# Grams, the product with the state, and the outputs of a delta-rule attention, issued by 32 stationary columns instead of 64

## The reference, cut to what matters

```
k_n = k / (norm(k) + 1e-6)            # B, H, S, D = 4, 8, 768, 48
for t in range(S):
    y[t]  = q[t] @ state
    v_old = state^T k_n[t]
    state = state + beta[t] * outer(k_n[t], v[t] - v_old)
x = y as (3072, 384)
h  = ((x @ w1) * (x @ w2)) @ w3 @ w_out     # inner width 1024
e  = h @ w_in                               # 384 -> 1024
s  = e * softmax(e);  out = layernorm(s) * g_ln @ w_out2
```

## Time and profile before

| | |
|---|---|
| time, median of 3 runs | 772.83 us (772.46 to 775.34) |
| time of the profiled execution | 774.38 us |
| its span, first to last instruction | 772.7 us |
| PE busy | 741.6 us (96%) |
| PEld / DVE / ACT / POOL busy | 664.5 / 451.2 / 339.5 / 66.6 us |
| granted TensorE clock | 0.999 of full speed |

### The profile page before, as it was taken

One profiled execution on the slowest core, in us unless ns is written; L12 is line 12 of the kernel. 1 busy time (PEld: TensorE's weight loads), 2 busy tenths in 40 slices (PEclk: granted clock), 3 DMA queues, 4 the chain that ended last, 5 costly groups with the idle time before them and its releaser, 6 DMA issues.

```text
span 772.7 us, 21207 instructions
## 1 busy us (share of the span) xinstructions
PE 741.6 (96%) x9012; PEld 664.5 (86%) x9012; DVE 451.2 (58%) x759; ACT 339.5 (44%) x704; POOL 66.6 (9%) x97
## 2 busy tenths in 40 slices
PE   7998898999999999899999999999999999999997
PEld 6666698998899899899999988888899999999987
DVE  1974973984695498378522444442456666656663
ACT  5636326333534433544244434443444444444443
POOL 2333200110020020002000000000000001000000
PEclk9999999999999999999999999999999999999999
DMA  9980360153036035104111494540000000000001
GB/s 260 322 260 13 102 180 21 41 148 95 24 95 168 17 87 149 56 30 118 43 37 43 164 285 151 160 140 1 0 22 23 22 22 23 23 20 20 21 22 31
DMA packets 41898, 66.87 MB, mean 87 GB/s; under 512 B 4312, under 2 KB 26968, under 8 KB 41816
## 3 DMA queue, kind: packets, MB, share of 16 engines
q1 hardware_dynamic: 38648, 59.00, 26.3%
q10 hardware_dynamic: 3168, 6.65, 2.6%
HBM read 46.76 MB, written 18.87 MB: 85 GB/s over the span
## 4 chain that ended last, share of the span: by engine, by line
PE 80%; DVE 9%; ACT 6%; issue 4%; DMA 2%; DVEq 0%
PE ps L1472 19%; PE ps L542 13%; PE ps L506 13%; PE ps L519 12%; PE ps L1376 5%; PE ps L1485 4%; ACT gd L1196 3%; PE ps L1388 3%; PE ps L531 3%; DVE kqs L918 2%; PE ps L1430 2%; ACT a L1204 2%; PE ps L1441 2%; PE ps L1360 1%; PE ps L1405 1%
## 5 line engine op out<-in xcount | busy, mean ns | idle before, releaser
L1264 ACT COPY asb<-ps 128x256 f32<-128x256 f32 x96 | 35.7, 372 | 151.4 <-PE ps L1472 150.6
L1078 DVE TENSOR_TENSOR msb<-asb,ps 128x256 f32<-128x256 f32 x96 | 39.7, 414 | 71.2 <-ACT asb L1264 66.7
L918 DVE TENSOR_TENSOR kqs<-ps,mask 64x512 f32<-64x512 f32 x48 | 33.0, 687 | 73.3 <-ACT a L1204 72.8
L542 PE MATMUL ps<-woh,uth 128*128 128x384 f32 x192 | 64.8, 337 | 0.5 <-DVE utl L459 0.5
L542 PE MATMUL ps<-woh,utl 128*128 128x384 f32 x192 | 64.5, 336 | 0.0
L542 PE MATMUL ps<-wol,uth 128*128 128x384 f32 x192 | 64.3, 335 | 0.0
L1472 PE MATMUL ps<-xh,w1h 128*128 128x256 f32 x288 | 57.4, 308 | 6.2 <-DVE msb L1078 6.2
L459 DVE TENSOR_TENSOR utl<-ps,uth 128x512 fp32r<-128x512 f32 x48 | 31.1, 686 | 48.2 <-ACT uth L349 48.2
L335 ACT ACTIVATE e<-ps,stats 128x1024 f32<-128x1024 f32 x24 | 26.8, 1116 | 67.3 <-DVE stats L425 67.3
L506 PE MATMUL ps<-mh,w34h 128*128 128x512 f32 x144 | 56.0, 389 | 0.0
L506 PE MATMUL ps<-ml,w34h 128*128 128x512 f32 x144 | 56.0, 389 | 0.0
(11 more groups left out here) (157 smaller groups left out, 1621.1 us busy)
## 6 DMA issues: line engine op xcount, KB each, us to landing
m_dram<-msb SPq DMA_DIRECT2D x42, 256.0 KB, 2.1
mrest<-m_dram SPq DMA_DIRECT2D x36, 256.0 KB, 5.8
kqs<-in_kq SPq DMA_DIRECT2D x20, 256.0 KB, 7.0
kqs<-in_kq SPq DMA_DIRECT2D x24, 192.0 KB, 5.7
vs<-in_vtok SPq DMA_DIRECT2D x6, 768.0 KB, 10.2
ks<-in_ktok SPq DMA_DIRECT2D x5, 768.0 KB, 6.2
mfirst<-m_dram SPq DMA_DIRECT2D x12, 256.0 KB, 6.1
out<-wst SPq DMA_DIRECT2D x12, 192.0 KB
```

The costliest lines, as they stand in the source:

```text
L542: ins = pe.matmul(ob[s], xx[:, j, k, :], w[:, 4 * j + k, :], start=(j == 0 and k == 0 and p == 0), stop=(j == 1 and k == 3 and p == 2))
L918: ins = dve.tensor_tensor(kqs[r, par, tile, 1 + bb, :, :], bank[r], mask[r, tile % NP, :].unsqueeze(1).to_broadcast([C, H, C]), ALU.mult)
L1078: dve.tensor_tensor(msb[:, f // 2 % 2, f % 2, :], asb[:, f % 2, :], bbank[f % 2], ALU.mult).then_inc(product, 1)
L1264: act.copy(asb[:, f % 2, :], abank[f % 2]).then_inc(a_kept, 1)
```

## The change

- `gbank` becomes two buffers, bank 2 and bank 3, each 8 heads by 64. The gram of a tile is split in two: `key_gram` (K^T K) and `query_gram` (K^T Q). Both are issued by halves of 32 stationary columns, at the PSUM partitions of `half_rows(bb, g, half)`, so four column groups. `key_gram` of the first half moves 64 columns, of the second only the last 32.
- `k_state` and `outputs` are issued by halves of 32 stationary columns too.
- Since each half of the keys lands where its rows are wanted, the diagonal block lies in columns 0 to 31 for all partitions: `keep_diagonal` is one copy of 128 partitions in place of four, the corner is in columns 32 to 63. `kqs` becomes `kt` (keys) and `z` (stacks of P and queries); keys and queries are loaded by separate DMAs with separate semaphores, in natural order of the tokens; the result is stored by one DMA a tile in place of one or four (60 become 24).
- `keep_pt` waits for the query gram, no longer behind ACT's copies.
- Order on PE: key grams 0 and 1 where gram 0 stood, key grams 2 and 3 where grams 1 and 2 stood, query grams 0 and 1 after fill 3; query grams 2 and 3 after fill 0 of the second chunk. On DVE the masks of tiles 0 and 1 stand together behind `system_rows`, those of 2 and 3 in the second chunk, after its products 0 and 2.

```diff
-        gbank = ps[:, 2:4, :].rearrange("p b (h c) -> p (b h) c", c=P)
+        gbank = [ps[:, 2 + j, :].rearrange("p (h c) -> p h c", c=C) for j in range(NP)]
...
-            def grams(n, tile):
...
-                pe.wait_ge(gram_kept, i)
-                pe.wait_ge(pt_made, i if i > TPG else 2)
...
-                        ins = pe.matmul(gbank[u_rows(bb), h, :], kqs[r, par, tile, 0, h, :],
-                                        kqs[r, par, tile, 0:2 + bb:1 + bb, h, :], start=True, stop=True)
+            def key_gram(par, tile, bank):
+                for h in range(H):
+                    for half in range(2):
+                        for bb in range(2):
+                            r, at = state_rows(bb), HB * half
+                            ins = pe.matmul(bank[half_rows(bb, tile % NP, half), h, 0:C - at],
+                                            kt[r, par, tile, h, at:at + HB], kt[r, par, tile, h, at:C],
+                                            start=True, stop=True)
+                ins.then_inc(gram, 1)
+            def query_gram(par, tile, bank):
...
+                            ins = pe.matmul(bank[half_rows(bb, tile % NP, half), h, :],
+                                            kt[r, par, tile, h, at:at + HB], z[r, par, bb, tile, h, :],
+                                            start=True, stop=True)
+                ins.then_inc(p_gram, 1)
+            def next_key_gram(n, tile):
+                i = TPG * (n + 1) + tile
+                pe.wait_ge(kt_in[(n + 1) % 2][tile // 2], 32 * ((n + 2) // 2))
+                if tile >= NP:
+                    pe.wait_ge(gram_kept, i + 1 - NP)
+                elif n == 0:
+                    pe.wait_ge(pt_made, tile + 1)
+                else:
+                    pe.wait_ge(x_low, i - TPG - 1)
...
+            def next_query_gram(n, tile):
+                i = TPG * (n + 1) + tile
+                pe.wait_ge(q_in[(n + 1) % 2][tile // 2], 32 * ((n + 2) // 2))
+                if tile < NP:
+                    pe.wait_ge(gram_kept, i + 1 + NP)
+                else:
+                    pe.wait_ge(x_low, i + 1 - TPG - NP)
...
             def k_state(n, par, tt, g):
-                        ins = pe.matmul(chain[g][u_rows(bb), hc(h)], kqs[r, par, tile, 0, h, :],
+                            ins = pe.matmul(chain[g][half_rows(bb, g, half), hc(h)], kt[r, par, tile, h, at:at + HB],
...
             def outputs(n, par, tt, g):
+                pe.wait_ge(pt_made, TPG if n == 0 else q + 1)
...
-                        ins = pe.matmul(chain[g][u_rows(bb), hc(h)], kqs[r, par, tile, 1 + bb, h, :],
-                                        us[r, g, bb, hc(h)], start=True, stop=True)
+                        for half in range(2):
+                            at = HB * half
+                            ins = pe.matmul(chain[g][64 * bb + at:64 * bb + at + HB, hc(h)],
+                                            z[r, par, bb, tile, h, at:at + HB],
+                                            us[r, g, bb, hc(h)], start=True, stop=True)
...
             def transpose_y(n, tt, g, ahead):
-                if tt == 0 and ahead:
-                    pe.wait_ge(gram_kept, TPG * (n + 2))
-                    pe.wait_ge(pt_made, TPG * (n + 2))
+                if ahead:
+                    pe.wait_ge(pt_made, q + TPG + 1)
...
-                for bb in range(2):
-                    for half in range(2):
-                        rows = slice(64 * bb + HB * half, 64 * bb + HB * (half + 1))
-                        ins = act.copy(gd[rows, tile * H:(tile + 1) * H, :],
-                                       gbank[rows, :, HB * half:HB * (half + 1)])
-                ins.then_inc(gd_kept, 1)
+                act.copy(gd[:, tile * H:(tile + 1) * H, :], bank[:, :, 0:HB]).then_inc(gd_kept, 1)
```

More of the change, by code:

```diff
@@ L45, with deltanet_moe_kernel @@
                       defaults=(None, None, None))
-def deltanet_moe_kernel(nc, kq, ktok, vtok, beta, w1, w2, w3t, wo1, win, wo2, gln, out):
+def deltanet_moe_kernel(nc, keys, queries, ktok, vtok, beta, w1, w2, w3t, wo1, win, wo2, gln, out):
     out_rows = out.rearrange("(b s) n -> b s n", b=B)
@@ L636, in flat, with pair @@
             return view.rearrange("p a h c -> p (a h c)").rearrange("p (c n) -> p c n", n=P)
-        w3s = [flat(kqs[:, 1, t, 0:2, :, :]) for t in range(TPG)]
+        def pair(view):
+            return view.rearrange("p t h c -> p (t h c)").rearrange("p (c n) -> p c n", n=P)
+        w3s = [pair(t[:, 2 * tt:2 * tt + 2]) for tt in range(2) for t in (kt[:, 1], z[:, 1, 0])]
         w3s += [flat(a21[:, 1, :, :, :]), w3raw[:, 0, :, :], w3raw[:, 1, :, :],
@@ L773, in load_kq @@
                 for bb in range(2):
[L774 to L777, removed]
+                    sp.dma_start(kt[state_rows(bb), n % 2, 2 * tt:2 * tt + 2, :, :],
+                                 keys[n, bb, :, tt]).then_inc(kt_in[n % 2][tt], 16)
+                for bb in range(2):
+                    sp.dma_start(z[loaded_rows(bb), n % 2, bb, 2 * tt:2 * tt + 2, :, :],
+                                 queries[n, bb, 0:D + 16 * bb, tt]).then_inc(q_in[n % 2][tt], 16)
             def load_k(n):
@@ L1187, in scale_first_v, with keep_diagonal @@
                 ins.then_inc(v_first, 1)
-            def keep_diagonal(n, tile, gbank):
+            def keep_diagonal(n, tile, bank):
                 act.wait_ge(gram, TPG * n + tile + 1)
@@ L1355, in tensor @@
         def tensor(pe):
-            def first_grams(part, tile, bank, done):
+            def key_gram(par, tile, bank):
                 for h in range(H):
[L1358 to L1362, removed]
-            def grams(n, tile):
-                par = n % 2
-                i = TPG * n + tile
-                pe.wait_ge(kq_in[par][tile // 2], 64 * ((n + 1) // 2))
-                pe.wait_ge(gram_kept, i)
-                pe.wait_ge(pt_made, i if i > TPG else 2)
-                if tile == 0 and n >= 2:
-                    pe.wait_ge(x_low, i - TPG)
-                pe.sem_inc(pe_passed, 1)
-                for h in range(H):
-                    for bb in range(2):
-                        r = state_rows(bb)
-                        ins = pe.matmul(gbank[u_rows(bb), h, :], kqs[r, par, tile, 0, h, :],
-                                        kqs[r, par, tile, 0:2 + bb:1 + bb, h, :], start=True, stop=True)
-                ins.then_inc(gram, 1)
@@ L1509, in group @@
                     if early and n > 0:
-                        grams(n + 1, 0)
+                        for tile in range(NP):
+                            next_key_gram(n, tile)
+                    if ahead and tt == 1:
+                        for tile in range(NP, TPG):
+                            next_query_gram(n, tile)
                     if tt == 0:
@@ L1514, in group @@
                     if early and n == 0:
-                        grams(n + 1, 0)
+                        for tile in range(NP):
+                            next_key_gram(n, tile)
                     fill(tt, 1)
                     if early:
-                        grams(n + 1, 1)
+                        next_key_gram(n, 2)
                     cross_half(n, par, tt)
@@ L1521, in group @@
                     if early:
-                        grams(n + 1, 2)
+                        next_key_gram(n, 3)
                     fill(tt, 3)
+                    if early:
+                        for tile in range(NP):
+                            next_query_gram(n, tile)
                     apply_inverse(n, par, tt, 1, rhs2, u2_done)
-                    if early:
-                        grams(n + 1, 3)
                     fill(tt, 4)
@@ L1542, in tensor @@
                 pe.wait_ge(k_first[tile // 2], 32)
-                first_grams(0, tile, first_a[tile], gram)
+                key_gram(0, tile, first_a[tile])
             for half in range(2):
@@ L1583, in lay_out @@
     return {
-        "kq": np.pad(np.stack([columns(k), columns(q)], axis=5), [(0, 0), (0, 0), (0, 64 - D)] + [(0, 0)] * 4),
+        "keys": columns(k),
+        "queries": np.pad(columns(q), [(0, 0), (0, 0), (0, 64 - D)] + [(0, 0)] * 3),
         "ktok": tokens(k),
```

126 lines of the change are left out of this document (63 added, 63 removed).

## The result

Slower: 807.38 us (median of 4; 804.51 to 809.77) against 774.09 us for the kernel before, a ratio of 1.0419, 95% interval 1.0363 to 1.0476. The profiled execution of the changed kernel took 807.42 us, its span is 805.7. The forecast of 747 and its range of 740 to 766 both missed, and the sign was wrong.

A forecast was written before the change was run, and what follows sets the result against it. PE bounds the kernel, busy 741.6 of 772.7 us. Outputs -5.7, k_state -4.2, grams +1.0, gram waits -13.3, fill waits -2.4 and -1.4 sum to -26.0: from 774.38 to 748.4, at the median 747 us; range 740 to 766.

The forecast's parts named there:

- What a small matmul costs: PE's small blocks: tiles on the same rows overlap, so doubled narrower pairs give outputs -5.7, k_state -4.2, grams +1.0 us.
- R1: Rival, outputs: four tiles on the same rows share their feed, 1.44 us a block, +8.1 us, 761 us; chance 0.15.
- R4: Rival, all small blocks: 32-column tiles on one row group run one after the other, 849 us; chance 0.13.
- Waits of the grams: PE's 13.3 us of gram waits for DVE's masks go, and nothing is late in their place.
- R3: Rival: waits change hands, grams waiting for ACT or transposes for masks; the 15.7 us stay, 763 us; chance 0.05.
- Waits of the fills, and the second chunk's cover: Fill waits for DVE's product: -2.4 us in first chunks, -1.4 in the first group's second; DVE fits 26.7 of 28.1 us.
- R2: Rival: DVE bounds the second chunk, half to all of 13.8 us given back, 754 to 761 us; chance 0.09.
- The chunks: Lengths by stretch: a first chunk from 38.6 to 32.7 us, a second one from 27.1 to 28.1 us.
- The sum: All terms of the whole kernel together: -26.0 us, from 774.38 to 748.4, given as 747 us at the median.
- M: Experiments' rival: the number or kind of matmuls stalls PE, by way of its array or its reads; no chance given.
- P: Experiments' rival: the new order or the two gram banks stall PE; no chance given.
- C: Experiments' rival: several tiles on the same rows, new with the 32-column outputs, are a hazard that stalls PE; no chance given.

The follow-up runs named there:

- e1: The change with its order, two gram banks and split grams kept, but all blocks at 64 stationary columns again; 770.21 us, ratio 0.9945 to the kernel before.
- e7: e1 with the key and query grams spread out among the fills, one at a time; 761.79 us, ratio 0.9834 to the kernel before.
- e8: The changed kernel with its grams spread out among the fills as in e7; 808.01 us, ratio 1.0426 to the kernel before.
- e5: The changed kernel with 38 warm-up matmuls in place of 6, so all code comes 64 pairs later; 818.65 us in one run.
- e6: The kernel before, with each product with the inverse issued twice (1536 more pairs); 794.64 us, ratio 1.0242 to the kernel before.
- e4: The changed kernel with loads of keys, queries, k and v for groups 2 to 5 cut to one partition; 787.24 us, ratio 1.0153 to the kernel before.
- e9: e7 with 3072 semaphore increments that nobody waits for among the fp32r matmuls of the fills; 1012.32 us.
- e10: e7 with 6144 semaphore increments that nobody waits for among the fp32r matmuls of the fills; 1556.96 us.
- e11: e7 with the outputs alone by 32 columns (768 more pairs); 768.11 us, ratio 0.9928 to the kernel before.

## Why the prediction was wrong

By its own steps:

- **What a small matmul costs**: right. Outputs 0.82 us (0.81 taken), k_state 1.51 (1.62), two query grams 1.92 (1.94). Four tiles on the same rows do run beside each other, 12.8 ns a pair in the outputs where two gave 33.4. R1 (1.44 us) and R4 (2.14 us) are both out.
- **Waits of the grams**: right. The changed kernel has no gram waiting for masks, nor for ACT, and neither have e1 and e7, where next to no stalls give the other engines time; R3 is out. ACT's four copies became one of 372 ns.
- **Waits of the fills, and the second chunk's cover**: right in groups 1 to 4, whose four waits of 0.6 us are gone in e7 too; DVE is busy 25.6 us of the second chunk from 229 to 260 us (26.7 were forecast) and holds nothing up. R2 is out. In the first group the number is luck. 4.1 of 6.2 us are gone, where 3.8 were taken, but ahead of the late product stands a stall of 5.29 us (to 94.14 us), which gives DVE the time; without it, in e7, a fill waits 2.9 us there (at 89.75 us; 2.8 in e1), more than the 2.47 of before, of which 1.4 were to go.
- **The chunks**: without their stalls, the first chunks of groups 1 to 4 last 33.4 to 34.3 us (32.7 forecast, 38.4 to 38.6 before) and the second ones 28.5 to 28.9 (28.1 forecast). Three of the four first chunks hold 3.4 us at the lower clock.
- **The sum**: this step failed, in what it left out. It priced the doubled pairs on PE's array and took that each is there to be issued. It put the sign of the change into the cost of a pair; the sign lay in 7296 more instructions of code. In its place the runs show 49.4 us of stalls, each until its own block of code is there. No rival had them. The row was on the page that I read first: 66 packets of instructions, against a PE that does 128 pairs in some 7 us before (a group of 38.6 + 27.1 us has 663 + 535 = 1198 pairs by the earlier trace rows, 9.4 blocks). The change has 384 + 256 = 640 more pairs a group, 14.4 blocks, and in the 61 us forecast for it that is one in 4.2 us on average; but where its small blocks stand together, 127 pairs take under 3 us (19 times, the table behind e8). Stalls follow each other at 3.5 us (124.36 to 127.90) to 5.9 us (214.39 to 220.24) a block.
- **R4's bound** priced twice as many pairs at the old pace and gave 849. The result lies between it and the forecast, but by another mechanism.

The account of the spans: 772.7, less 17.4 of waits (13.3, and 6.2 - 2.1), less 10.3 of work (k_state 11 x 0.49, outputs 22 x 0.25, grams + 0.6), plus 49.2 of stalls (49.4, less 0.2 before) gives 794.2. Without the stalls these terms come to 27.7 us, where the forecast had 26.0, the luck in the first group among them. A further 8.1 us is in the fills: their six forms sum to 307.8 us busy before and 315.9 after. This goes with the clock. It was 0.999 on average before and 0.978 now. Up to 470 us the changed kernel has seven stretches at the lower level, 31 us in all, and six of them begin in a stall or within 1.1 us of its end; the kernel before has none between 17 and 772 us. Windows around the stall of 4.53 us at 12.93 us and the one of 6.08 us at 39.49 us (length; busy PE, PEld, DVE, ACT, POOL; granted clock):

```profile
10.00:16.00 6.00, 3.07 (x48) 2.26 (x48) 1.19 (x1) 1.63 (x5) 0.00 (x0) 0.75 1.03 275
36.00:46.00 10.00, 6.51 (x105) 4.81 (x105) 9.85 (x7) 1.16 (x3) 8.32 (x6) 0.66 0.71 229
```

0.75 and 0.66 of full speed are mixtures of the two levels, 2.4 and 1.2 GHz. That leaves 3.4 us of 805.7 unaccounted.

What is shown: the stalls come at fixed distances in the code, not in the work (e5); they are there with old blocks alone (e6), they go with the code (e1, e7), and they shrink when data loads do (e4). And in the ten kernels of the first table and e5, all 148 stalls of 0.15 us or more end 1.2 to 1.7 us after a packet has landed, and it is each time the packet of the block at whose border PE stands. An array or an instruction that stalled by itself (M, P, C) would not end its stalls there. What stays open: code could not be added without time (e9, e10), so its share apart from the pairs was not measured; and why a packet starts as late as 4.8 us after PE has reached the block before it is told only in part by the data loads (15 of 80 packets over 2 us in the change, 7 of 81 in e4).

## What to carry to other kernels

Where a change multiplies small instructions on an engine with a long unrolled program, price its code as well. Take the instruction packets and the time that each packet's instructions last, before and after, and look at the densest stretches, not at the mean: here a packet's worth of pairs in under 3 us stalled 35 times of 38 (the change and e8), and one of 5 us or more hardly ever. Splitting a matmul into narrower tiles can be free or better on the array and still lose. What paid here was the other part of the change, two buffers for the grams and a shorter chain behind them, with as few pairs as possible (e7, 1.7% faster).

## What was not expected of the hardware

- Code comes to PE in portions of about 252 instructions, by the packets, with stalls of 0.2 to 6.1 us at their borders. Two packets never started less than 3.3 us apart in any of these kernels, though one takes 1.1 us. The stalls came up between 9652 pairs (0.8 us in e7, 4.0 in e1) and 10420 (10.4 us, e11), and traffic of data lengthens them.
- A semaphore increment among the fp32r matmuls of the fills costs PE 82 ns with two behind each matmul (e9), and (1556.96 - 761.79) / 6144 = 129 ns with four (e10), where the granted clock was near the lower level through most of the attention, 0.681 on average over the span:

```profile
PE   8988998888988899888898988989899999999997
...
PEclk9955555565565655656556555565655799999999
```

- Four tiles of 32 columns on the same 112 or 128 rows run at 12.8 ns a pair with 48 fp32 columns moving, as fast as four tiles with rows of their own (12.7).
